# Fifteen block products for eighteen in a pair of hidden tiles, with finished tiles kept in PSUM

## The reference

```python
# first: 4 experts, all evaluated for each token; p is normalised over the experts
for e in range(4):
    h = np.maximum(x @ w1[e], 0.0)          # 384 -> 1024
    out += p[:, e:e + 1] * (h @ w2[e])      # 1024 -> 384
# second, on x = out
h = x @ w_in                                # 384 -> 2048
g = h * (1.0 / (1.0 + np.exp(-1.702 * h)))
return g @ w_out                            # 2048 -> 384
```

## Time and profile before

| | us |
|---|---|
| median of the runs | 642.7 (642.1 to 642.85) |
| span of the profiled execution, first to last instruction | 640.5 |
| TensorE busy in it | 635.2 |
| VectorE, ScalarE, GpSimd busy | 222.4, 203.4, 170.0 |

### The profile page before, as it was taken

One profiled execution on the slowest core, in us unless ns is written; L12 is line 12 of the kernel. 1 busy time (PEld: TensorE's weight loads), 2 busy tenths in 40 slices (PEclk: granted clock), 3 DMA queues, 4 the chain that ended last, 5 costly groups with the idle time before them and its releaser, 6 DMA issues.

```text
span 640.5 us, 9440 instructions
## 1 busy us (share of the span) xinstructions
PE 635.2 (99%) x3880; PEld 529.3 (83%) x3880; DVE 222.4 (35%) x369; ACT 203.4 (32%) x421; POOL 170.0 (27%) x168
## 2 busy tenths in 40 slices
PE   8999999999999999999999999999999999999998
PEld 6999888888888888888888888888888888888886
DVE  8987642212121212121212121213533333333332
ACT  4744432332222212222211223223643333333223
POOL 5664300342242303242402245422750000000000
PEclk9999999999999999999999999999999999999999
DMA  8765521006000501000310000220000010001001
GB/s 331 278 217 189 202 115 51 4 1 247 1 0 1 196 2 49 2 0 1 151 47 1 0 1 0 98 101 1 2 0 1 3 47 1 0 2 50 1 0 50
DMA packets 8722, 39.08 MB, mean 61 GB/s; under 512 B 1504, under 2 KB 1632, under 8 KB 7392
## 3 DMA queue, kind: packets, MB, share of 16 engines
q1 hardware_dynamic: 8672, 38.40, 15.9%
HBM read 36.01 MB, written 2.38 MB: 60 GB/s over the span
## 4 chain that ended last, share of the span: by engine, by line
PE 98%; DVE 1%; DMA 0%; issue 0%; ACT 0%; DVEq 0%
PE bank L1097 46%; PE bank L1123 31%; PE bank L1139 15%; PE bank L1171 2%; PE bank L1215 1%; PE bank L1218 1%; PE bank L1205 1%; PE bank L1190 1%; PE bank L1208 0%; DMA wu_sb<-wu_rows 0%; DVE w_pow L800 0%; DVE q_k_mid L816 0%; PE bank L1223 0%; DVE q_tab_k L807 0%; DVE acc L951 0%
## 5 line engine op out<-in xcount | busy, mean ns | idle before, releaser
L1097 PE MATMUL bank<-x_hi,w_hi 128*128 128x512 f32 (+1 forms) x456 | 172.5, 378 | 0.0
L1097 PE MATMUL bank<-x_lo,w_hi 128*128 128x512 f32 (+1 forms) x456 | 172.4, 378 | 0.0
L1097 PE MATMUL bank<-x_hi,w_lo 128*128 128x512 f32 (+1 forms) x456 | 172.3, 378 | 0.0
L876 DVE SCALAR_TENSOR_TENSOR h_lo<-bank,h_hi 128x512 fp32r<-128x512 f32 (+1 forms) x104 | 67.5, 649 | 257.3 <-ACT h_hi L700 257.3
L700 ACT ACTIVATE h_hi<-bank 128x512 fp32r<-128x512 f32 (+1 forms) x104 | 58.7, 564 | 286.6 <-PE bank L1097 286.6
L622 POOL TENSOR_TENSOR w_lo<-staging,w_hi 128x384 fp32r<-128x384 f32 x80 | 82.2, 1039 | 173.4 <-ACT w_hi L670 173.4
L1123 PE MATMUL bank<-h_hi,w_hi 128*128 128x512 f32 (+1 forms) x312 | 117.7, 377 | 0.1
L1123 PE MATMUL bank<-h_hi,w_lo 128*128 128x512 f32 (+1 forms) x312 | 116.3, 373 | 0.0
L1123 PE MATMUL bank<-h_lo,w_hi 128*128 128x512 f32 (+1 forms) x312 | 116.3, 373 | 0.0
L1097 PEld LDWEIGHTS bank<-x_hi,w_hi 128*128 128x128 f32 x456 | 85.8, 188 | 15.9
L1097 PEld LDWEIGHTS bank<-x_hi,w_lo 128*128 128x128 f32 x456 | 85.8, 188 | 15.8
(11 more groups left out here) (86 smaller groups left out, 433.4 us busy)
## 6 DMA issues: line engine op xcount, KB each, us to landing
staging<-weights SPq DMA_DIRECT2D x10, 1536.0 KB, 8.7
rkv_in<-rkv_n SPq DMA_DIRECT2D x10, 640.0 KB, 5.5
rk_in<-rk_t SPq DMA_DIRECT2D x12, 512.0 KB, 5.2
staging<-weights SPq DMA_DIRECT2D x4, 768.0 KB, 8.9
p_bc<-p_normalised SPq DMA_DIRECT2D x4, 768.0 KB, 4.2
out<-p_bc SPq DMA_DIRECT2D x9, 256.0 KB, 2.1
rkv_in<-rkv_n SPq DMA_DIRECT2D x2, 448.0 KB, 5.7
u_bc<-u_rows SPq DMA_DIRECT2D x1, 192.0 KB, 11.7
```

Source lines behind the costliest of these rows:

```text
L876: dve.scalar_tensor_tensor(h_lo[:, slot, 0:size], hid, 0.0, h_hi[:, slot, 0:size].bitcast(F32), ALU.max, ALU.subtract).then_inc(sem["hlo"], 1)
L1097: last = pe.matmul(bank[:, HID[j % 2], 0:tokens.stop - tokens.start], w[:, k, :], xs[c][:, k, tokens], start=(n == 0), stop=(n == 3 * KT - 1))
```

## The change

From expert 1 on, two neighbouring hidden tiles form a pair: 2 x 3 weight blocks times 3 x 3 blocks of x, 18 block products. They are replaced by 15 products of sums of weight blocks (a_hi, a_lo) with blocks of x or sums of them (s_hi, s_lo, eight sums). PRODUCT lists for each its weight, its rows, its bank (LEFT or RIGHT), whether it begins the bank's sum anew, whether its bank is copied (take, ScalarE, to a temporary) or joined (VectorE, bank plus or minus the temporary), the result, and the sign. So a bank is read between two products that both go on summing in it. A result's last join writes to one of two PSUM banks (OVER). There VectorE's gate works in place: maximum with 0 times the probability in the experts, times the sigmoid in the second network. ScalarE's high part and VectorE's low part follow. A group is the output for one token block n and row block k, both tiles, six passes; two of the nine stay in their own banks over all the pairs of a network (KEPT), the others use two banks in turn (SHARED) and leave, added by VectorE to acc, in every pair. The probability now stands at the tile, and GpSimd's gather is gone: its steady work is sums and low parts of weights.

There are 20 pairs. Pair 12 (PLAIN), the first of the second network, has its six tiles as nine-pass products as before, while x is formed anew from acc. `form` makes the eight row sums by 13 two-input VectorE instructions in place: for expert 1 during the last steps of expert 0, for the second network behind the plain tiles. Each engine follows one list, ordered by the positions in PLACES, in passes from the start of a pair's products; pair 0's positions are pressed into its 45 passes, since it has no groups among its products. Positions (at) order an engine's list and are no times.

```diff
+MIXED, AFTER_PLAIN = (1, 2, 2, 2, 2, 2, 2, 0, 2, 0), (0, 0, 0, 0, 0, 2, 1, 2, 2, 8)
+TAKES = {"product": 3, "group": 6, "plain": 9}
+STRETCH = 99
+PLACES = (
+    {"take": (4, 16, 28, 37, 49, 63), "join": (15, 25, 40, 53, 67, 76, 79, 91, 100), "gate": (43, 57, 73, 85, 97, 109),
+     "high": (47, 60, 79, 89, 100, 112), "low": (50, 64, 82, 94, 106, 117), "leave": (12, 22, 34, 46, 60, 70, 103)},
+    {"take": (4, 14, 26, 35, 47, 59), "join": (12, 26, 38, 50, 65, 74, 80, 90, 100), "silu": (42, 55, 69, 84, 93, 105),
+     "gate": (47, 62, 77, 87, 97, 115), "high": (53, 66, 81, 90, 100, 119), "low": (59, 71, 84, 94, 106, 122),
+     "leave": (9, 20, 32, 44, 56, 68, 103)},
+)
...
+LEFT, RIGHT = 5, 6
+PRODUCT = (
+    (2, (1, 0), LEFT, True, "copy", 0, 1),
+    (10, (0, 0), LEFT, True, "add", 0, 1),
+    (0, (1, 1), RIGHT, True, "copy", 1, 1),
+    (12, 8, LEFT, False, "add", 1, -1),
+    (9, 13, RIGHT, True, "copy", 4, 1),
+    (7, 3, LEFT, False, "copy", 2, 1),
+    (11, (2, 1), RIGHT, False, "add", 1, 1),
+    (4, (0, 2), LEFT, False, "copy", 5, 1),
+    (13, 14, RIGHT, False, "add", 0, -1),
+    (8, 9, RIGHT, False, "copy", 3, -1),
+    (1, 4, LEFT, False, "add", 4, -1),
+    (14, 10, RIGHT, False, "add", 5, -1),
+    (6, (2, 2), LEFT, True, "add", 5, -1),
+    (3, 1, LEFT, False, "add", 3, -1),
+    (5, (1, 2), RIGHT, False, "add", 2, -1),
+)
...
+FORMED = {3: ((0, 2), 3), 8: ((1, 1), 4), 4: ((0, 1), 5), 13: ((2, 1), 8), 14: ((2, 0), 9), 9: ((1, 0), 10), 10: ((1, 2), 12), 1: ((0, 0), 13)}
+FORMINGS = 13
+ROWS_AT = {JOIN + 1: (0, 1), JOIN + 2: (2, 3, 4), JOIN + 3: (5, 6, 7)}
...
+LAST_OF = {row[5]: i for i, row in enumerate(PRODUCT)}
+DONE = sorted(range(6), key=lambda o: LAST_OF[o])
...
+        KEPT, SHARED, OVER = (0, 1), (3, 4), (2, 7)
+        PLAIN_BANKS = (5, 6, *OVER)
...
+            order = [("product", 0, i) for i in range(PRODUCTS)]
+            def mix(q, lead):
+                left = iter(range(PRODUCTS))
+                for n, takes in enumerate(lead):
+                    if n:
+                        order.append(("group", q, *GROUPS[n - 1]))
+                    order.extend(("product", q + 1, next(left)) for _ in range(takes))
+            for q in range(ALL_PAIRS - 1):
+                if q == PLAIN - 1:
+                    order += [("group", q, *what) for what in GROUPS[:6]] + [("plain", PLAIN, i) for i in range(2)]
+                    order += [("group", q, *what) for what in GROUPS[6:]] + [("plain", PLAIN, i) for i in range(2, 6)]
+                elif q == PLAIN:
+                    mix(q, AFTER_PLAIN)
+                else:
+                    mix(q, MIXED)
+            order += [("group", ALL_PAIRS - 1, *what) for what in GROUPS]
...
+            for t in range(-2, ALL_PAIRS):
+                if 2 <= t + 4 < ALL_PAIRS:
+                    sp.wait_ge(sem["alo"], PARTS_W[t + 3])
+                    load_first(t + 4)
+                if t == -2:
+                    sp.wait_ge(sem["slo"], len(SUM_ORDER))
+                    load_probs(1)
+                    sp.wait_ge(sem["ev1"], KT * len(SPANS))
+                    load_probs(2)
+                if 2 <= t + 3 < ALL_PAIRS:
+                    sp.wait_ge(sem["vlo"], t + 2)
+                    load_second(t + 3)
+                if t == PAIRS_E - 1:
+                    sp.wait_ge(sem["gate"], 6 * PAIRS_E)
+                    load_probs(3)
...
+            def sum_low(turn, blocks, i):
+                op = SUM_ORDER[i]
+                pool.wait_ge(sem["shi"], len(SUM_ORDER) * turn + i + 1)
+                pool.tensor_tensor(sum_home(s_lo, x_lo, op), blocks[FORMED[op][0]], sum_home(s_hi, x_hi, op).bitcast(F32),
+                                   ALU.subtract).then_inc(sem["slo"], 1)
...
+            def sum_high(turn, blocks, i):
+                op = SUM_ORDER[i]
+                block, formed = FORMED[op]
+                act.wait_ge(sem["form"], FORMINGS * turn + formed)
+                if turn == 0:
+                    act.wait_ge(sem["xlo"], CH)
+                    act.wait_ge(sem["l1"], MEET)
+                else:
+                    act.wait_ge(sem["prod"], PRODS[PLAIN + 1])
+                act.activation(sum_home(s_hi, x_hi, op), blocks[block], ACT.Copy).then_inc(sem["shi"], 1)
...
+            def take(q, i):
+                _, _, at, _, _, o, sign = PRODUCT[i]
+                number = t_number(q, o)
+                act.wait_ge(sem["prod"], PRODS[q] + i + 1)
+                if number >= T_RING:
+                    act.wait_ge(sem["added"], t_before(number))
+                act.activation(t_of[number % T_RING], bank[:, at, :], ACT.Copy, scale=float(sign)).then_inc(sem["copied"], 1)
...
+            def tile_high(q, pos):
+                number = 6 * q + pos
+                if number >= H_RING:
+                    act.wait_ge(sem["grp"], tile_before(number))
+                act.wait_ge(sem["gate"], number + 1)
+                act.activation(tile_hi[number % H_RING], over_bank(q, pos), ACT.Copy).then_inc(sem["thi"], 1)
...
+                for i in ROWS_AT.get(j, ()):
+                    sum_high(0, blocks0, i)
+                if j == STEPS - 2:
+                    for piece in range(3):
+                        weight_high(0, piece)
+            for piece in range(3, len(PIECES)):
+                weight_high(0, piece)
+            second_high(0)
...
+            def join(q, i):
+                _, _, at, _, _, o, sign = PRODUCT[i]
+                t = t_of[t_number(q, o) % T_RING]
+                before = [x for x in ADDED if x < i and PRODUCT[x][5] == o]
+                dve.wait_ge(sem["prod"], PRODS[q] + i + 1)
+                if before:
+                    dve.wait_ge(sem["added"], JOINED[q] + ADDED.index(before[-1]) + 1)
+                else:
+                    dve.wait_ge(sem["copied"], TAKEN[q] + COPY_OF.index(o) + 1)
+                new = t
+                if LAST_OF[o] == i:
+                    pos = DONE.index(o)
+                    new = over_bank(q, pos)
+                    if q == 0:
+                        dve.wait_ge(sem["ev1"], KT * len(SPANS))
+                    if 6 * q + pos >= len(OVER):
+                        dve.wait_ge(sem["tlo"], 6 * q + pos - len(OVER) + 1)
+                if sign > 0:
+                    dve.tensor_tensor(new, bank[:, at, :], t, ALU.add).then_inc(sem["added"], 1)
+                else:
+                    dve.scalar_tensor_tensor(new, bank[:, at, :], -1.0, t, ALU.mult, ALU.add).then_inc(sem["added"], 1)
+            def leave(q, n, k):
+                i = LEAVES[q, n, k]
+                cols = slice(n * NB, (n + 1) * NB)
+                dve.wait_ge(sem["grp"], groups(q, n, k))
+                src = bank[:, KEPT[k] if kept(n, k) else shared_bank(q, n, k), :]
+                if q < MOE_PAIRS:
+                    if q and not kept(n, k):
+                        dve.wait_ge(sem["evac"], LEAVES[q - 1, n, k] + 1)
+                    else:
+                        dve.wait_ge(sem["ev1"], KT * len(SPANS))
+                    dve.tensor_tensor(acc[:, k, cols], src, acc[:, k, cols], ALU.add).then_inc(sem["evac"], 1)
...
+            def tile_gate(q, pos):
+                over = over_bank(q, pos)
+                if q < MOE_PAIRS:
+                    o = result_of(q, pos)
+                    e, cols = 1 + q // PAIRS_E, slice(o % 3 * NB, (o % 3 + 1) * NB)
+                    dve.wait_ge(s_prob[e % 2], 16 * (e // 2 + 1))
+                    dve.wait_ge(sem["added"], final(q, o))
+                    dve.scalar_tensor_tensor(over, over, 0.0, p_of[e % 2][:, cols], ALU.max, ALU.mult).then_inc(sem["gate"], 1)
+                else:
+                    number = 6 * (q - MOE_PAIRS) + pos
+                    dve.wait_ge(sem["silu"], number + 1)
+                    dve.tensor_tensor(over, over, part[:, number % 2, :], ALU.mult).then_inc(sem["gate"], 1)
+            def tile_low(q, pos):
+                number = 6 * q + pos
+                dve.wait_ge(sem["thi"], number + 1)
+                dve.tensor_tensor(tile_lo[number % H_RING], over_bank(q, pos), tile_hi[number % H_RING].bitcast(F32),
+                                  ALU.subtract).then_inc(sem["tlo"], 1)
...
+                if j == JOIN:
+                    dve.wait_ge(sem["xlo"], CH)
...
+                    for k, n in ((1, 1), (0, 2), (2, 1), (2, 2), (1, 2)):
+                        cols = slice(n * NB, (n + 1) * NB)
+                        dve.tensor_tensor(blocks0[k, n], x_hi[:, k, cols].bitcast(F32), x_lo[:, k, cols].bitcast(F32),
+                                          ALU.add).then_inc(sem["blockv"], 1)
                 step(j)
+                if j == JOIN:
+                    dve.wait_ge(sem["block"], 4)
+                    dve.wait_ge(sem["blockv"], 5)
+                    for i in range(0, 5):
+                        form(0, blocks0, i)
+                elif j == JOIN + 1:
+                    for i in range(5, 10):
+                        form(0, blocks0, i)
```

(49 more changed lines are left out.)

641 lines of the change are left out of this document (424 added, 217 removed).

## The result

The changed kernel takes 641.4 us (median of 20 runs, 639.4 to 642.6) against 642.4 (642.1 to 642.9, 20 runs); the ratio is 0.9978, 95% interval 0.9970 to 0.9986. So it is faster by 0.2%, about 1 us (less than the 1.3 us that the prediction named as the least it could tell from no change), where 14.5 us were forecast, and the time is outside the range of 615 to 638. The profiled execution has a span of 639.9 us where the prediction's sum gave 626.0: 13.9 us have to be found. The first two lines are from the page of the changed kernel, the busy times (against the earlier trace rows) and the granted clock in 40 slices of 16 us.

The account below looks back on a forecast made before the run. TensorE, busy 99% of the span, was taken as the bound. Span 640.5 - 38.8 + 0.1 + 24.2 (boundary stalls) = 626.0 us; with 2.2 carried over to the median, 628.2 us, range 615 to 638.

Parts of the forecast that it names:

- Removed passes and steady pairs: From expert 1 on, 171 passes go, 38.8 us; a steady pair lasts 99 passes, 22.4 us, without stall.
- rival of leaking pairs: Steady pairs lose 0.3 to 0.5 us in each of 18, giving 633 to 637; chance 0.24 up to 641.4.
- dear writes to PSUM: Rival: VectorE's gates and last joins pay extra writing PSUM; 646 us at 0.4 us each; chance 0.04.
- 0 to 0.04 that was kept: Extra time allowed for each VectorE instruction that writes PSUM: 0 to 0.04 us.
- Boundary 1: Expert 0's last tokens, forming row sums: a stall of 2.8 us plus 0.3 for GpSimd, 3.1 in all.
- 0.3 for GpSimd: Expert 0's end: GpSimd's low parts run beside VectorE's last three sums; 0 to 0.7 us, 0.3 taken.
- Boundary 2: Pair 0, without output groups between products: the bare chain of banks, gates and low parts costs 8.2 us.
- Boundary 4: The last nine groups: group 4 waits for the last tile's low part, 8 passes or 1.8 us.
- the wait at the start of boundary 3: Behind pair 11's products the fourth group waits for tile 5's low part, 8.85 passes.
- Boundary 3: Around the plain pair: waits of 42.25 passes, 9.6 us, plus 1.5 us for contention with GpSimd; 11.1 in all.
- 1.5 for GpSimd: Around the plain pair: two VectorE sums slowed by GpSimd's row low parts, 1.5 us (0 to 4 for all 13).
- rival of the clock: Broken-up products at pair 0 and around the plain pair fall to 1.2 GHz; about 645 us, chance 0.03.

Follow-up runs that it names:

- nowait: Changed kernel with ScalarE's row-sum conversions in expert 0's last steps waiting for hidden pass 23 instead of 27; 639.3 us, ratio 0.9953.
- all3: nowait, pair1_late, leaves_scalar, rows_vector and meet_late together, last tiles' steps earlier, pair 0's low parts reordered, expert 0's row low parts on VectorE; 623.0 us, ratio 0.9695.
- weights_late: Changed kernel with pair 14's weight sums behind the eight row sums and its weight conversions behind pair 13's copies; 635.0 us, ratio 0.9889.
- forms_early: Changed kernel with VectorE's 13 row sums around the plain pair 24 clock units (list positions) earlier; 641.0 us, ratio 0.9971.
- filler: Changed kernel with eleven additional TensorE passes, results unused, put into the wait at 127.8 us; 641.2 us, ratio 0.9970.
- rows_late: Changed kernel with the eight row sums of expert 0's last steps put two steps later (27 to 29); 642.6 us, ratio 1.0001.
- pair1_late: weights_late with pair 1's five weight conversions also later, behind the copies that pair 0's products wait for; 634.4 us, ratio 0.9874.
- leaves_scalar: weights_late with the six evacuations of pair 12's groups on ScalarE instead of VectorE; 633.9 us, ratio 0.9876.
- meet_late: nowait with TensorE's branch ending three hidden passes later, behind hidden pass 30 instead of 27; 639.4 us, ratio 0.9957.
- rows_vector: leaves_scalar with the eight row low parts around the plain pair on VectorE instead of GpSimd; 632.1 us, ratio 0.9841.

## Why the prediction was wrong

- **Removed passes and steady pairs: right.** 22.44 us a pair with TensorE never idle. The rival of leaking pairs fell, and so did that of dear writes to PSUM. VectorE's instructions that write PSUM, by line and form (busy us, mean ns, idle before):

```profile
L1422 DVE SCALAR_TENSOR_TENSOR bank<-bank,t_most 128x512 f32<-128x512 f32 x95 | 65.8, 693 | 15.2 <-PE bank L1809 13.7
L1422 DVE SCALAR_TENSOR_TENSOR t_most<-bank,t_most 128x512 f32<-128x512 f32 x38 | 26.0, 684 | 2.1 <-PE bank L1809 2.1
```

  0.693 us into PSUM against 0.684 into SBUF: within the 0 to 0.04 that was kept.
- **Boundary 1: the wait right (2.76 for 2.8), two terms missing.** 1.75 us of slow passes, and 0.79 at 123.56, where a low part stood behind VectorE's sums; the first of these began 2.28 us after the instruction before it (named issue), behind the end of VectorE's own branch. That the branch's end made it late is argued: no run moves that end. The "0.3 for GpSimd" does not show as a wait in this kernel; in nowait there was one of 1.26 us, and it went when all3 took the row low parts off GpSimd.
- **Boundary 2: right in size (8.8 for 8.2).** One wait had another cause (a take behind pair 1's weights), but taking it away gave 0.5 us, since the named chain ends almost as late.
- **Boundary 4 and the wait at the start of boundary 3: right** (1.93 for 1.8; 1.9 for 2.0), and with the last tile's steps put first the one at the end went and the other fell to 0.9.
- **Boundary 3: the step that failed, 22.2 for 11.1.** The prediction laid out TensorE's, VectorE's and ScalarE's lists there, and cost GpSimd only as contention ("1.5 us"). It never asked when GpSimd's weight sums for pair 14 would come, with eight row low parts among them and the whole in a pair shortened to 69 passes; in ScalarE's strict order each late sum holds a take. The two waits are 5.5 us, and weights_late removed them. The clock, which was a rival at 0.03 and not a term, fell twice there, and only one fall cost time. That of 450 to 460 cost nothing (weights_late). That behind the second take cost 2.3 us: the changed kernel lost 7.0 us from there on, and nowait and forms_early, whose clock stayed up there, lost 4.7 each.

  Some 3.3 us are left, and the starts of the passes show where: 1.4 at the evacuations (5.3 for the 2.4 of the three groups and the 1.5 for GpSimd), 0.55 at 441.43 (named issue) and 0.6 at 464.09, at places where no wait was forecast, 0.5 in pair 13's last products, and the rest in pieces of 0.1. Six of VectorE's sums took 1.16 to 1.77 us, 3.9 more in sum than at 0.68 each, inside the stated bound of 4: two of them (1.6) stand at the evacuations, as charged, and four (2.3) behind 457.9, ahead of the join for which the product at 464.09 waits. What made the first evacuation late, at 450.47, is open.
- **The rival of the clock** had the mechanism right and its extent wrong: not all the broken-up products, but the passes behind waits of 2 us and more, and of these falls only some cost time. The Trainium skill's section on depth-cycling, cited there, tells of small idle times; here waits of 0.2 to 1.8 us in pair 0 left the clock at full. The size of a fall could not be foretold from the wait: 2.76 us was followed by nine slow passes, 2.71 us (475.23) by fourteen, and 2.1 us (450.47) by several in the changed kernel and by none in weights_late. Falls also differ from execution to execution, and with them the time: of the changed kernel's 20, those with a mean clock of 0.995 or more took 639.4 to 640.1 us, those at 0.989 to 0.992 took 640.7 to 642.6.

So of 14 us, the runs show one cause: GpSimd's queue seen through ScalarE's. Putting pair 14's weights later gave 7.1 us, which is 5.5 of waits and 2.3 of the slow passes behind them, less what came back. That TensorE's idleness brings the clock down is shown too (filler), but at boundary 1 that gave no time, since a wait at the branch's end took its place; there only the edits together did, 4.1 us at pair 0's start in all3. What stays open is the late first evacuation, the 0.55 us at 441.43, and whether the branch's end costs TensorE something in every run.

## What to carry to other kernels

Where engines take their work strictly in order, lay out every queue at a boundary, the slowest engine's first: an operation that is needed now must not stand behind one that waits for an engine with a backlog. A long wait can cost more than itself, since TensorE's next passes may run at half speed; but slow passes cost time only where TensorE is what the others wait for, so look at the starts behind them and not at the clock alone. Two engines' work on SBUF in the same stretch is worth a row of its own in the sum. A gain taken at one boundary is kept only when the next one has room: here four single edits (rows_late, filler, pair1_late, leaves_scalar) gave back most of what they won. And before a gain of 1 or 2 us is put down to an edit, see that the trace has it at the place that was edited: nowait's ratio is 1.6 us better than the changed kernel's, and 0.5 us of it were its own.

## What was not expected of the hardware

- Behind 2.76 us without work nine passes ran 0.427 us apart and then full speed returned, and the clock fell at this place in all six traces with this wait; with filling passes in it no pass was slow.
- The first instruction behind the end of a branch came 2.28 us after the one before on VectorE, and 1.2 to 1.7 us late on TensorE in rows_late, filler and nowait, named issue; with the branch ending three hidden passes later (meet_late) TensorE lost nothing.
- A VectorE sum of two SBUF tensors took up to 1.79 us beside GpSimd (leaves_scalar), for 0.68 alone (rows_vector), 2.6 times as long.
